# Attention and two expert layers in one kernel: where the first half's transposes stand in a one-tile slot

## What is computed

```python
# attention: 4 x 8 heads, 576 positions, width 64; scores below (row maximum - tau) are dropped
scores = scale * q @ k.T
scores = where(scores >= max(scores) - tau, scores, -1e9)
x = softmax(scores) @ v                       # heads side by side: (2304, 512)
# experts with routing: 8 experts, one for each token
e = argmax(x @ w_gate)
y[token] = gate[token] * (relu(x[token] @ w1[e]) @ w2[e])     # w1: 512 x 1024, w2: 1024 x 512
# experts without routing: 4 experts, all tokens through each, weighted by p
out = sum over e of p[:, e] * (relu(y @ v1[e]) @ v2[e])
```

## Time and profile before

| what | us |
|---|---|
| median of three runs | 1392.14 (1388.88 to 1392.37) |
| the profiled execution | 1389.17 |
| its span, first to last instruction | 1387.4 |
| TensorE busy | 1370.3 (99% of the span) |
| VectorE busy | 989.1 (71%) |
| ScalarE busy | 672.5 (48%) |
| GpSimd busy | 181.6 (13%) |
| mean granted TensorE clock | 0.999 |

### The profile page before, as it was taken

One profiled execution on the slowest core, in us unless ns is written; L12 is line 12 of the kernel. 1 busy time (PEld: TensorE's weight loads), 2 busy tenths in 40 slices (PEclk: granted clock), 3 DMA queues, 4 the chain that ended last, 5 costly groups with the idle time before them and its releaser, 6 DMA issues.

```text
span 1387.4 us, 27887 instructions
## 1 busy us (share of the span) xinstructions
PE 1370.3 (99%) x10213; PEld 1201.3 (87%) x10213; DVE 989.1 (71%) x1491; ACT 672.5 (48%) x1164; POOL 181.6 (13%) x330
## 2 busy tenths in 40 slices
PE   8999999998999999999999999999999999999999
PEld 7777777777888888899898989989898989989897
DVE  7888888865877777798766757784766687584762
ACT  6777777764666666665322324442332444142320
POOL 3222222213122222251000000200000020000000
PEclk9999999999999999999999999999999999999999
DMA  4332323214988889943131212311130322111111
GB/s 94 68 70 58 67 61 70 54 27 137 350 279 279 284 293 304 351 139 110 59 106 32 105 61 77 137 61 65 57 106 32 121 80 88 61 62 64 57 61 46
DMA packets 170165, 160.67 MB, mean 116 GB/s; under 512 B 89808, under 2 KB 122672, under 8 KB 170096
## 3 DMA queue, kind: packets, MB, share of 16 engines
q1 hardware_dynamic: 163072, 140.65, 32.4%
q0 software_dynamic: 5824, 18.83, 3.8%
q10 hardware_dynamic: 1200, 0.26, 0.1%
HBM read 143.58 MB, written 16.12 MB: 115 GB/s over the span
## 4 chain that ended last, share of the span: by engine, by line
PE 95%; DVE 2%; issue 1%; ACT 1%; DMA 0%; POOL 0%; ACTq 0%; DVEq 0%; POOLq 0%
PE front L1249 6%; PE front L1248 6%; PE front L1247 6%; PE back L834 6%; PE back L1177 6%; PE back L1178 6%; PE back L1179 6%; PE front L859 4%; PE front L1119 3%; PE front L1117 3%; PE front L1118 3%; PE back L1248 3%; PE back L1249 3%; PE back L1247 3%; PE front L877 2%; PE front L1179 2%
## 5 line engine op out<-in xcount | busy, mean ns | idle before, releaser
L1177 PE MATMUL back<-x2h,w1h 128*128 128x384 f32 x480 | 160.8, 335 | 0.2 <-DVE two L1966 0.2
L1179 PE MATMUL back<-x2h,w1l 128*128 128x384 f32 x480 | 160.5, 334 | 0.0
L1178 PE MATMUL back<-x2l,w1h 128*128 128x384 f32 x480 | 160.4, 334 | 0.0
L1249 PE MATMUL front<-dn_h,h2l 128*128 128x512 f32 x384 | 149.8, 390 | 0.0
L1248 PE MATMUL front<-dn_l,h2h 128*128 128x512 f32 x384 | 149.7, 390 | 0.0
L1247 PE MATMUL front<-dn_h,h2h 128*128 128x512 f32 x384 | 149.6, 389 | 0.0
L1525 ACT COPY one<-front 128x384 f32<-128x384 f32 x48 | 22.6, 470 | 206.8 <-PE front L1179 189.0
L789 POOL DMA_INDIRECT out<-rows,out_i x15 | 20.0, 1332 | 698.2 <-DVE rows L1958 696.3
L834 PEld LDWEIGHTS back<-vv,pt 128*64 128x64 f32 x2840 | 89.3, 137 | 13.1 <-issue 13.1
L834 PE MATMUL back<-vv,pt 128*64 128x65 f32 x2840 | 100.2, 224 | 0.0
L1841 DVE TENSOR_TENSOR w1l<-w1r,w1h 128x1024 fp32r<-128x1024 f32 x84 | 97.5, 1216 | 0.0
(11 more groups left out here) (298 smaller groups left out, 3622.0 us busy)
## 6 DMA issues: line engine op xcount, KB each, us to landing
early<-in_moe_w SPq DMA_DIRECT2D x64, 512.0 KB
ring<-in_moe_w SPq DMA_DIRECT2D x64, 512.0 KB
w1r<-in_moe_w SPq DMA_DIRECT2D x48, 512.0 KB, 3.8
dn_r<-in_moe_w SPq DMA_DIRECT2D x48, 512.0 KB, 5.8
tokens_x<-x_nat SPq DMA_DIRECT2D x16, 288.0 KB, 4.4
vv<-in_v SPq DMA_DIRECT2D x32, 128.0 KB, 2.3
raw<-in_k SPq DMA_DIRECT2D x30, 128.0 KB, 2.7
raw<-in_q SPq DMA_DIRECT2D x30, 128.0 KB, 2.6
```

The lines of the kernel that those rows point to most:

```text
L1177: pe.matmul(to[:, 0:CH], w1h[:, w, kk, fs], x2h[:, x, kk, :], start=start and kk == 0, stop=False, skip_group_check=not start)
L1178: pe.matmul(to[:, 0:CH], w1h[:, w, kk, fs], x2l[:, x, kk, :], start=False, stop=False, skip_group_check=not start)
L1179: last = pe.matmul(to[:, 0:CH], w1l[:, w, kk, fs], x2h[:, x, kk, :], start=False, stop=kk == 1, skip_group_check=not start)
L1249: last = pe.matmul(to, h2l[:, f, ts], w2_block(dn_h, f), start=False, stop=n == KF - 1)
```

## The change

In a single slot the transposes of the first half are no longer made in the middle of the second half's products, but behind all 24 products and ahead of the next tokens' transposes. ScalarE takes the two ReLUs one after the other, and then the two casts.

```diff
@@ up_single(m, g), TensorE
                     for kk in range(KD):
-                        if a == 1 and kk == 2:
-                            turn_h(m, 0)
                         pe.matmul(S[0][:, a, :], xch[:, kk, 0:P], w1_half(up_h, kk, a), start=kk == 0, stop=False)
@@ slot(m, b), TensorE
                     up_single(m, j)
                 else:
                     up(j, j, n * P)
+                if single(m, b):
+                    turn_h(m, 0)
                 if final(m, b):
                     first_rows()
                 else:
@@ slot(m, b), ScalarE
                     relu_rows(j, 0)
+                    relu_rows(j, 1)
                     rows_hi(m, 0)
-                    relu_rows(j, 1)
                     rows_hi(m, 1)
```

## The result

The changed kernel takes 1393.95 us (median of 18 runs, 1391.76 to 1396.95), the kernel before 1390.46 us (median of 18 runs beside them, 1388.60 to 1392.80). The ratio is 1.0026, with a 95% interval of 1.0020 to 1.0032: slower by about 3.6 us, clearly measured, and within the 0.3% that the prediction counted as no change. The predicted step was 3.2 us.

The account below looks back on a forecast made before the run. The prediction took TensorE, busy 99% of the span, as the bound. Seven single slots at 0.45 us made 3.2 us, put on the 1392.14 us median of three runs: 1395.3 us, range 1391.0 to 1397.5.

Parts of the forecast that it names:

- the 0.3%: Whole kernel: a measurement can tell about 0.3%, 4.2 us, from no change; the forecast step was 0.23%.
- What bounds it: Routed-expert layer, 360 to 622 us: TensorE busy 262.00 of 262.00 us, so no idle time can swallow a delay.
- The move of TensorE's work by itself: TensorE in single slots: if nothing waited, the move would gain 0.01 to 0.10 us per slot, under 0.7 in all.
- a rival counted as a bubble: No wait: mixing products and transposes costs a break (0.32, not 0.23), which the change removes; 1391.4 to 1392.1 us, chance 0.16.
- The chain: Single slot: transposes, cast, VectorE's rest, then the second layer's first load; costs 0.45 us per slot, seven times, 3.2 us.
- by a hair: First half's cast on ScalarE: transposes allow it at 0.93 us after the first layer's last product starts, the ReLU at 0.91.
- the slower rival: ScalarE's cast may not overlap the ReLU ahead of it: 0.16 us more per slot, 4.3 us in all, 1396.4; chance 0.20.
- The size: Seven single slots: 0.45 us each, 3.2 us in all.
- The restart: TensorE starting again after the late load: no extra taken, 0.11 us per slot (0.8 us) as upper bound.
- The rival that the clock falls: TensorE's clock drops in single slots after 16 transposes in a row plus the wait: 1407 us, chance 0.02.
- The time: Whole kernel: 1395.3 us, the step put on the 1392.14 median of three runs.
- their waits move with TensorE: DMA, GpSimd and SyncE issue the same instructions; costed at nothing, covered by 24 products, 5.5 us.

Follow-up runs that it names:

- late_rest: Changed kernel, single slot's second layer begun with four products that need only the first half's cast, those reading VectorE's rest behind them: ratio 0.9993 to the kernel before.
- act_swap: Kernel before with only ScalarE's order changed, the second half's ReLU ahead of the first half's cast, TensorE's order as before: ratio 1.0041.
- pe_move: Changed kernel with ScalarE's old order back, first half's cast ahead of the second half's ReLU, so only TensorE's transposes moved: ratio 1.0028 to the kernel before.
- split_rest: Changed kernel with VectorE's rest of the first half in two instructions of two blocks each: ratio 1.0009 to the kernel before.
- tokens_first: Changed kernel with the eight token transposes ahead of the first half's four: ratio 1.0074 to the kernel before.
- hold_before: Kernel before with GpSimd's four weight mixes held until VectorE's first down-weight rest of the last pair slot is done: ratio 1.0001.

## Why the prediction was right, point by point

- **What bounds it.** TensorE without idle time from the first slot on, so that every delay is paid. Right: the seven waits of 0.42 each come out as 3.0 us in the profile, and nothing swallows them: from its first product to the end of the span, the second expert part takes 752.0 us in both profiles.
- **The move of TensorE's work by itself: nothing.** Right. `late_rest` has the new order without the wait and is as fast as before, 0.05 us per slot better. The 0.32 behind the transposes that a rival counted as a bubble is no loss of its own: from 507.96 to 508.63 is 0.67, which is four transposes of 0.109 and a product of 0.23.
- **The chain.** Four links, each from a row of the kernel before; the measured ones agree within 0.01 us (table above). One reading in it was finer than the runs bear out. The prediction let the transposes set the cast "by a hair"; the two causes tie. With the transposes long done (`act_swap`) the cast starts 0.49 behind the ReLU, at T + 0.92; with no ReLU in front (`pe_move`) it starts 0.69 behind the transposes, at T + 0.93. In the change both are met at T + 0.93 (511.24 to 511.73 is 0.49, 511.04 to 511.73 is 0.69), so either alone would put it there to within 0.01 us. That ScalarE overlaps the two although a wait stands between them was the point on which the slower rival hung; it does, and the rival fell.
- **The size.** 0.45 per slot was forecast, 0.42 measured by the spacing, 3.2 against 3.0 us. The rows and the spacings do not carry more.
- **The restart.** No extra was taken. From load to the second product it was 511.36 - 511.01 = 0.35 before, and it is 513.50 - 513.16 = 0.34 now. By the Trainium skill's rule that a load is pulled ahead of matmuls in flight (TensorE: Matmul & The Clock Gate, section "Step-by-step: what each phase is for") the old load was to be hidden and the new one not, 0.8 us more; here the row decided, rightly: the trace does not agree that this load was hidden. It issues 0.03 us ahead of its product, while the next one, at 511.12, issues 0.24 ahead of its own. The wait that stands on it is not the reason: in the old order the first load behind the first half's transposes, at 508.28, has no wait and also issues 0.03 ahead.
- **The clock.** Granted 1.00 from 360 to 622 us after as before, with sixteen transposes in a row and 0.45 us of standing still. The rival that the clock falls is out. The Trainium skill (same page, section "Part 4: PE-mode transpose") says that transposes do not count as busy for the clock in the way that matmuls do; whether or not, this row of sixteen did not bring it down here.
- **The time.** 1395.3 was forecast, 1393.95 measured, inside 1391.0 to 1397.5. Most of the 1.35 is the base: the median of the three runs at hand, 1392.14, lay 1.7 above the median of eighteen, 1390.46. The step itself, from that base, would have given 1393.7. Part of this closeness is luck: the measured step of 3.6 us holds the 3.0 of the slots and, going by the profiles, up to 1.0 of a cost that was not foreseen (next point).
- **Not foreseen.** The two waits in the last pair slot, 1.0 us of the profiled difference. The prediction costed GpSimd at nothing, "their waits move with TensorE". That step failed in this place: a moved phase between GpSimd and VectorE has a price although neither waits for the other by a semaphore. It did not turn the forecast, since 1.0 us is small against the 4.2 us of the 0.3%.

What stays open: in how many executions those two waits occur. Among the other profiles of kernels with moved slots, `act_swap` has one of them, and `pe_move`, `split_rest` and `tokens_first` have none. The long rest itself is there more often: 3.71 us in `act_swap` and 3.42 in `tokens_first`.

## What to carry to other kernels

- When work is moved from beside something to the end, count what is queued behind it until its first user, and compare it with the chain that it starts, link by link from start to start. Here, from the first transpose on, 1.7 us of cover met a chain of 2.1: the difference is the cost. In the old place, and also three products later, the chain ends ahead of the load and the cost is zero.
- Among pieces of equal cost put first the one that starts a chain, and the ones that serve only as cover behind it; and let a consumer wait for each operand where it is first used, not for all of them ahead of the first instruction.
- In a kernel whose stages repeat, measure by the spacing of the repeats in the trace. A few hundredths of a us per slot can be read there, where totals of different executions differ by 4 us.

## What the runs showed of the hardware that was not expected

- **VectorE and GpSimd disturb each other without a semaphore.** A VectorE subtraction of 128x1024 takes 1.21 us alone, 2.8 to 2.9 in the kernel before where it meets GpSimd's sums, and 4.15 in the changed kernel, where GpSimd's began 0.66 behind it. With GpSimd held until it was done, it took 1.29. In all eleven profiles the two engines' rows then end by turns: VectorE's 1.07 to 1.10 us behind the end of the GpSimd sum that it meets, and the next sum 2.25 to 2.29 behind that. The one exception is in `split_rest`, where the sum began 0.91 behind VectorE's row: that row took 1.23 and the sum 2.58. From the kernel before, where the sum ahead of these rows ends at 595.00 (their ends are 596.09 and 599.44, and 598.36):

```profile
593.24 2.85 DVE L1821 TENSOR_TENSOR dn_l<-ring,dn_h 128x1024 fp32r<-128x1024 f32 x1 [0.52 <-ACT dn_h L1410]
596.68 2.76 DVE L1821 TENSOR_TENSOR dn_l<-ring,dn_h 128x1024 fp32r<-128x1024 f32 x1
```

```profile
595.14 3.22 POOL L732 TENSOR_TENSOR w1r<-w1r 128x1024 f32<-128x1024 f32 x1
```

  The Trainium skill (SBUF — State Buffer, section "Who interferes with whom") says that a VectorE instruction with two SBUF inputs contends with a GpSimd instruction that reads SBUF, one blocking the other. The trace agrees, in both directions: a VectorE row of 2.85 has only its last 1.09 behind GpSimd's end, and a GpSimd row of 3.22 only its last 2.27 behind VectorE's. Being first by the listed start did not protect VectorE: its row of 4.15 starts 0.66 ahead of GpSimd's and still ends 1.09 behind it, while GpSimd's takes the 2.40 that it takes in the kernel before.
- **Profiled executions reach the first slot at different times.** TensorE's first product of the first slot starts at 339.37 us before, 339.39 after, 340.04 in `pe_move`, 341.43 in `act_swap`, 341.82 in `split_rest`, 342.91 in `hold_before` and 343.40 in `tokens_first`, though none of these kernels differs ahead of it. The profiled execution of `hold_before` took 1392.52 us, 3.35 more than the one of the kernel before, and it starts its first slot 3.54 later. A difference of 4 us between two profiled spans can be this alone, and it is as large as the effect studied here.
- **The granted clock ahead of the slots varies likewise.** It is 0.67 in the window 324 to 326 us before and 0.50 in the same window after, behind the same idle stretch from 319 to 321. From 321 us to the first slot it is 0.91 before and 0.72 after, with TensorE listed as busy for 14.08 and 16.66 us. Yet the first slot starts within 0.02 us in both. Late in this stretch TensorE waits for the first tokens from DMA, 2.2 us before and 0.4 us after, so the lower clock only used up idle time. The wait in the kernel before and in the changed one:

```profile
PE back L1059 <- DMA xst<-tokens_x,idx: 2.2, 1, 2.2
```

```profile
PE back L1059 <- DMA xst<-tokens_x,idx: 0.4, 1, 0.4
```
